# Second tiles' gate values moved from TensorE to VectorE, and first-pair operand splits moved behind the attention stage, in a fused attention and expert kernel

## What is computed

```
# 1 chunked attention: 8 heads of 64, chunks of 32 queries, each over 8 memory keys + up to 56 keys around it
a   = softmax(q_c @ k_full.T / 8);  x = a @ v_full
# 2 channel mix, with x_prev the row before
xk  = mu_k * x + (1 - mu_k) * x_prev;   xr = mu_r * x + (1 - mu_r) * x_prev
x2  = sigmoid(xr @ w_r) * (relu(xk @ w_k) ** 2 @ w_v)          # w_k 512x1024, w_v 1024x512, w_r 512x512
# 3 experts: logits of 8 experts and one local gate, row by row
logits = x2 @ w_gate;  local = sigmoid(x2 @ w_local)
e      = argmax(logits[s]) if s == 0 or local[s] < 0.5 else e of the row before
out[s] = softmax(logits[s])[e] * (relu(x2[s] @ w1[e]) @ w2[e])
```

## Time and profile before

| what | value |
|---|---|
| runs | 488.22, 488.89, 490.28 us, median 488.89 |
| profiled execution | 489.2 us, its span 487.6 us |
| mean granted TensorE clock | 0.945 |
| TensorE busy | 444.6 us (91%) |
| VectorE busy | 263.6 us (54%) |
| ScalarE busy | 222.2 us (46%) |
| attention stage | 0 to 74.56 us |
| six mix pairs | 74.56 to 261.4 us |
| rest of the routing | 261.4 to 283.4 us |
| expert slots | 283.4 to 487.6 us |

### The profile page before, as it was taken

How to read it: one execution, slowest core, us unless ns; L and a number is a source line. 1 busy time by engine, 2 the same in 40 slices (tenths; PEclk the granted TensorE clock), 3 DMA queues, 4 the chain that set the end, 5 groups by cost and what they waited for, 6 DMA issues and landing times.

```text
span 487.6 us, 9976 instructions
## 1 busy us (share of the span) xinstructions
PE 444.6 (91%) x3792; PEld 370.1 (76%) x3792; DVE 263.6 (54%) x596; ACT 222.2 (46%) x332; POOL 52.8 (11%) x70
## 2 busy tenths in 40 slices
PE   2686769999999999999999879999999999999991
PEld 2564558889898898988987667787777777777771
DVE  3577882355634656448494557223822374746851
ACT  1446652633636446354591145223622373727740
POOL 0001000000010100101001211112111111111110
PEclk9958557999999999999999989999999999999997
DMA  8889749825072270630911189311740166565610
GB/s 314 335 302 396 267 160 356 337 118 230 0 286 107 86 302 1 272 117 33 340 39 45 58 301 410 117 43 33 232 181 28 44 200 224 188 219 164 240 29 11
DMA packets 23729, 87.34 MB, mean 179 GB/s; under 512 B 3151, under 2 KB 3279, under 8 KB 23697
## 3 DMA queue, kind: packets, MB, share of 16 engines
q1 hardware_dynamic: 18048, 70.87, 39.4%
q0 software_dynamic: 5360, 16.04, 9.8%
q10 hardware_dynamic: 288, 0.02, 0.0%
HBM read 55.34 MB, written 32.62 MB: 180 GB/s over the span
## 4 chain that ended last, share of the span: by engine, by line
PE 82%; DMA 6%; DVE 4%; issue 3%; ACT 1%; POOL 0%; SPq 0%; POOLq 0%; ACTq 0%; DVEq 0%
PE PS L592 18%; PE PS L609 18%; PE PS L465 15%; PE PS L498 14%; PE PS L481 7%; PE PS L600 3%; PE PS L519 2%; PE PS L577 2%; DMA RAW<-wmix 1%; DMA VV<-tiles 1%; DMA QK<-tiles 1%; PE PS L418 1%; PE PS L509 1%; DMA CO<-consts 1%; PE PS L429 1%
## 5 line engine op out<-in xcount | busy, mean ns | idle before, releaser
L1100 DVE TENSOR_TENSOR EL<-ERAW,EH 128x1024 fp32r<-128x1024 f32 x56 | 66.5, 1217 | 2.7 <-ACT EH L797 2.6
L797 ACT ACTIVATE EH<-ERAW 128x1024 fp32r<-128x1024 f32 x56 | 57.6, 1056 | 11.3 <-PE PS L609 8.8
L465 PE MATMUL PS<-XHI,WHI 128*128 128x256 f32 x192 | 56.3, 293 | 0.9 <-issue 0.9
L1168 DVE TENSOR_TENSOR HL<-PS,HH 128x512 fp32r<-128x512 f32 x32 | 22.0, 690 | 64.8 <-ACT HH L811 64.8
L465 PE MATMUL PS<-XHI,WLO 128*128 128x256 f32 x192 | 54.8, 285 | 0.0
L465 PE MATMUL PS<-XLO,WHI 128*128 128x256 f32 x192 | 54.7, 285 | 0.0
L592 PE MATMUL PS<-EH,XSH 128*128 128x512 f32 x128 | 52.7, 412 | 1.4 <-DVE XSL L1106 1.4
L609 PE MATMUL PS<-EH,HH 128*128 128x512 f32 x120 | 51.0, 425 | 1.5 <-DVE EL L1100 0.6
L592 PE MATMUL PS<-EL,XSH 128*128 128x512 f32 x128 | 51.4, 401 | 0.0
L592 PE MATMUL PS<-EH,XSL 128*128 128x512 f32 x128 | 51.2, 400 | 0.0
L609 PE MATMUL PS<-EH,HL 128*128 128x512 f32 x120 | 47.3, 394 | 0.0
(11 more groups left out here) (157 smaller groups left out, 826.2 us busy)
## 6 DMA issues: line engine op xcount, KB each, us to landing
ERAW<-wexp SPq DMA_DIRECT2D x56, 512.0 KB, 5.7
expert_rows<-ZR SPq DMA_DIRECT2D x6, 4112.0 KB, 13.8
QK<-tiles SPq DMA_DIRECT2D x12, 768.0 KB, 6.8
VV<-tiles SPq DMA_DIRECT2D x12, 520.0 KB, 6.2
RAW<-wmix POOLq DMA_DIRECT2D x10, 512.0 KB, 6.0
XR<-expert_rows POOLq DMA_DIRECT2D x17, 257.0 KB, 3.2
CO<-consts SPq DMA_DIRECT2D x1, 340.0 KB, 6.2
rows_out<-OSB,OIDX POOLq DMA_INDIRECT x16, 5.3
```

Of the source, the lines that this page charges most:

```text
L465: last = nc.tensor.matmul(PS[q % 2][:, half * 256:half * 256 + 256], w[:, c:c + P], x[:, k, :], start=n == 0, stop=n == 11)
L797: nc.scalar.activation(expert_part(EH1, EH2, w, c), ERAW[c][:], ACT.Copy).then_inc(ehi_done, 1)
L1100: nc.vector.tensor_tensor(expert_part(EL1, EL2, w, c), ERAW[c][:], expert_part(EH1, EH2, w, c).bitcast(F32), ALU.subtract).then_inc(elo_do ...
L1168: nc.vector.tensor_tensor(HL[:, 4 * part:4 * part + 4, :].rearrange("p k n -> p (k n)"), PS[2 + part][:, :], HH[:, 4 * part:4 * part + 4, ...
```

## The change

Five things change.

1. The gate values (8 logits and the local gate) of the second tile of pairs 0 to 4 no longer come from TensorE. The nine weight columns are laid out as rows on the host (`wrows`), loaded once and copied to all partitions (`WGB`, nine tiles of 128 x 512), and VectorE's `products(p, part)` makes nine products with a sum over the row, three in each of three parts: before `squared(g, 0)`, before `squared(g, 1)` and before `squared(g, 2)`. TensorE loses four transposes and eight passes of `logits` in each of the pairs 1 to 5, ScalarE one `x2_out`, VectorE one `logits_out`. The last tile, t = 11, stays on TensorE.
2. Of the ten weight chunks 0 to 5 are split in the tiles 2, 3, 4, 5, 7 and 9 (`CHUNK_AT`), and chunks 6 to 9 (`w_v`) in pair 0, one behind each `relu_square` and `squared`. The load of chunk 6 waits for the values of tile 9.
3. Kind 1 of pair 0's inputs is built and split in `mix(0)`: `mix_scaled` and `mix_full` before the first `relu_square` and `squared`, `mix_hi` and `mix_lo` behind it.
4. SyncE's queue: the nine `WGB` loads stand behind the wait for all ten chunks and ahead of the zero writes, and the first expert's loads also wait until all of pair 4's products are made (`logit_evac` at 11), since `WGB` and `JUNK` lie in memory that is used again.
5. In `mix(5)` VectorE's `gated(5, 0)` stands ahead of `lo(5)`, `x_lo(0)` and `lo(6)`, no longer behind them.

```diff
+CHUNK_AT = {2: 0, 3: 1, 4: 2, 5: 3, 7: 4, 9: 5}
...
+        top[0] = inner + 2 * W2
+        JUNK = [X2T[1][:].rearrange("p k n -> p (k n)"), place("JUNK1", [P, D])[:]]
+        WGB = [place(f"WGB{e}", [P, D], at=(ring + KT * XTW + e * D if e < 4 else whi + N1 * CH1 + (e - 4) * D
+                                            if e < NE else wlo + N1 * CH1 + 2 * XGW + 4)) for e in range(NE + 1)]
... SyncE
+            sp.wait_ge(pv_done, NT)
+            sp.wait_ge(xt_done, NT)
             sp.wait_ge(wlo_done, N1)
+            for e in range(NE + 1):
+                sp.dma_start(WGB[e][:], wrows[e:e + 1, :].to_broadcast([P, D])).then_inc(wgb_loaded, 16)
...
             sp.wait_ge(xf_done[1], NPAIR)
+            sp.wait_ge(logit_evac, NT - 1)
             for c in SPLIT0:
                 expert_load(x, c)
... TensorE, mix
                 up(g, 0, first)
                 if not first:
-                    logits(2 * g - 2, 0, g - 1)
-                    x2_transposed(2 * g - 1, 1 if odd else 3, False)
+                    logits(2 * g - 2, g - 1, 0, g - 1)
                 up(g, 1, first)
-                if not first:
-                    logits(2 * g - 1, 1, g - 1)
... ScalarE
-                if t >= 2:
-                    weight_hi(t - 2)
-                if t in (6, 7):
-                    mix_scaled(0, t - 6, True)
-                if t in (8, 9):
-                    mix_hi(0, t - 8, True)
+                if t in CHUNK_AT:
+                    weight_hi(CHUNK_AT[t])
+                if t == 6:
+                    mix_scaled(0, 0, True)
+                if t == 8:
+                    mix_hi(0, 0, True)
...
             def mix(g, first, last):
-                if not first:
-                    x2_out(2 * g - 2, 0)
+                if first:
+                    mix_scaled(0, 1, True)
+                else:
+                    x2_out(g - 1, 0)
                 relu_square(g, 0, first)
-                if not first:
-                    x2_out(2 * g - 1, 1)
+                if first:
+                    mix_hi(0, 1, True)
+                    weight_hi(len(CHUNK_AT))
                 for q in range(1, 4):
                     relu_square(g, q, first)
+                    if first:
+                        weight_hi(len(CHUNK_AT) + q)
... VectorE (the attention tiles as on ScalarE)
+            def products(p, part):
+
+                t = 2 * p + 1
+                dve.wait_ge(wgb_loaded, 16 * (NE + 1))
+                dve.wait_ge(x2_done, t + 1)
+                for e in range(3 * part, 3 * part + 3):
+                    n = p * (NE + 1) + e
+                    if n >= 2:
+                        dve.wait_ge(product_done, n - 1)
+                    last = nc.vector.scalar_tensor_tensor(JUNK[n % 2], X2F[:, t % 4, 0:D], 1.0, WGB[e][:], ALU.mult,
+                                                          ALU.mult, accum_out=LG[:, t, e:e + 1])
+                    last.then_inc(product_done, 1)
+                if part == 2:
+                    dve.wait_ge(product_done, (p + 1) * (NE + 1))
+                    dve.sem_inc(logit_evac, 1)
...
+                if first:
+                    mix_full(0, 1, True)
+                else:
+                    products(p, 0)
                 squared(g, 0, first)
-                if not first:
-                    logits_out(2 * p)
+                if first:
+                    mix_lo(0, 1, True)
+                    weight_lo(len(CHUNK_AT))
+                else:
+                    logits_out(2 * p, p)
+                    products(p, 1)
                 squared(g, 1, first)
-                if not first:
-                    logits_out(2 * p + 1)
+                if first:
+                    weight_lo(len(CHUNK_AT) + 1)
+                else:
+                    products(p, 2)
                 squared(g, 2, first)
                 if first:
+                    weight_lo(len(CHUNK_AT) + 2)
...
                 squared(g, 3, first)
+                if first:
+                    weight_lo(len(CHUNK_AT) + 3)
...
+                if last:
+                    gated(g, 0, False)
                 lo(5)
                 if last:
                     x_lo(0, PS[1])
                     lo(6)
-                gated(g, 0, first)
+                else:
+                    gated(g, 0, first)
... GpSimd
+                if n == len(CHUNK_AT):
+                    pool.wait_ge(pv_done, NT - 2)
                 pool.dma_start(RAW[n % 2][:], wmix[:, n * CH1:(n + 1) * CH1]).then_inc(raw_loaded[n % 2], 16)
```

More of the change, by code:

```diff
@@ L54, with moe_program @@
 C_NF, C_POS, C_EXP, C_SLOT, CW = 508, 520, 584, 648, 808
+CHUNK_AT = {2: 0, 3: 1, 4: 2, 5: 3, 7: 4, 9: 5}
 SLAB = 52800
 FRESH_AT = -1.5 * 2.0 ** -23
-def moe_program(nc, tiles, wmix, mus, wgate, wexp, consts, out):
+def moe_program(nc, tiles, wmix, mus, wgate, wrows, wexp, consts, out):
     ctx = ExitStack()
@@ L219, in moe_program @@
         x2_done = sem("x2_done")
+        wgb_loaded = sem("wgb_loaded")
+        product_done = sem("product_done")
         x2t_done = sem("x2t_done")
@@ L501, in down, with x2_transposed @@
                     last.then_inc(down_done, 1)
-            def x2_transposed(t, at, first):
+            def x2_transposed(t, n, at, first):
                 pe.wait_ge(x2_done, t + 1)
                 if not first:
-                    pe.wait_ge(x2t_evac, t)
+                    pe.wait_ge(x2t_evac, n)
                 for k in range(KT):
@@ L511, in x2_transposed, with logits @@
                 last.then_inc(x2t_done, 1)
-            def logits(t, u, pairs):
-                pe.wait_ge(x2t_evac, t + 1)
+            def logits(t, n, u, pairs):
+                pe.wait_ge(x2t_evac, n + 1)
                 pe.wait_ge(logit_evac, t + 1)
@@ L561, in mix @@
                 if last:
-                    x2_transposed(2 * g, 2, False)
+                    x2_transposed(2 * g, g, 2, False)
                     down(g, 1, first, range(12, 18))
-                    logits(2 * g, 0, g)
+                    logits(2 * g, g, 0, g)
                     down(g, 1, first, range(18, 24))
@@ L567, in mix @@
                     down(g, 1, first, range(12, 24))
-                    x2_transposed(2 * g, 2 if odd else 0, first)
+                    x2_transposed(2 * g, g, 2 if odd else 0, first)
             def x_slot(s, bank):
@@ L630, in _ @@
             h_passes(0, 0, range(3))
-            x2_transposed(NT - 1, 3, False)
+            x2_transposed(NT - 1, NPAIR, 3, False)
             h_passes(0, 0, range(3, 7))
-            logits(NT - 1, 1, NPAIR - 1)
+            logits(NT - 1, NPAIR, 1, NPAIR - 1)
             h_passes(0, 0, range(7, 12)).then_inc(h_done, 1)
@@ L783, in sigmoid, with x2_out @@
                 nc.scalar.activation(SG[u][:], PS[2 + u][:, :], ACT.Sigmoid).then_inc(sig_done, 1)
-            def x2_out(t, u):
-                act.wait_ge(x2t_done, t + 1)
-                act.wait_ge(logit_done, t + 1)
+            def x2_out(n, u):
+                act.wait_ge(x2t_done, n + 1)
+                if u:
+                    act.wait_ge(logit_evac, NT - 1)
+                act.wait_ge(logit_done, n + 2)
                 nc.scalar.activation(X2T[u][:].rearrange("p k n -> p (k n)"), PS[6][:, :],
@@ L849, in _ @@
                 mix(g, g == 0, g == NPAIR - 1)
-            x2_out(NT - 2, 0)
-            x2_out(NT - 1, 1)
+            x2_out(NPAIR - 1, 0)
+            x2_out(NPAIR, 1)
             route_exps(NPAIR - 1)
@@ L967, in attention @@
                 normed(t, u, t < 2)
[L968 to L973, removed]
+                if t in CHUNK_AT:
+                    weight_lo(CHUNK_AT[t])
+                if t == 6:
+                    mix_full(0, 0, True)
+                if t == 8:
+                    mix_lo(0, 0, True)
             dve.wait_ge(const_in, 48)
@@ L1001, in squared, with logits_out @@
                                         ALU.subtract).then_inc(klo_done, 1)
-            def logits_out(t):
-                dve.wait_ge(logit_done, t + 3)
+            def products(p, part):
[12 more added lines that the diff above has]
+                    dve.sem_inc(logit_evac, 1)
+            def logits_out(t, n):
+                dve.wait_ge(logit_done, n + 3)
                 nc.vector.tensor_copy(LG[:, ds(t, 1), :].rearrange("p a n -> p (a n)"),
@@ L1011, in gated @@
                 dve.wait_ge(sig_done, t + 1)
-                if not first:
-                    dve.wait_ge(x2t_done, t - 1)
                 if g >= 2:
+                    if u == 0:
+                        dve.wait_ge(x2t_done, g - 1)
                     dve.wait_ge(rows_scattered, 32 * (g - 1))
@@ L1159, in mix @@
                 if last:
-                    logits_out(2 * g)
+                    logits_out(2 * g, g)
                 gated(g, 1, first)
@@ L1179, in _ @@
             tail = NPAIR - 1
-            logits_out(NT - 1)
+            logits_out(NT - 1, NPAIR)
             flags(tail)
@@ L1438 @@
```

(1 more changed line is left out.)

## The result

Four runs of the changed kernel took 481.45, 482.31, 482.78 and 483.42 us, median 482.54, against 488.79 for the kernel before: a ratio of 0.9866 with a 95% interval of 0.9836 to 0.9896. It is faster, by about half of what was forecast (476.6, range 472.5 to 482.0); the median lies just above the range. The profiled execution took 482.78, with a span of 481.2 us.

What follows compares the result with a forecast made beforehand. It took the mix pairs as bound by TensorE and attention by VectorE and ScalarE alternating. Terms -6.0 - 2.1 + 0.4 - 5.1 (pairs 1 to 4) + 0.5 = -12.3 took profiled 489.2 to 476.9, median 476.6; range 472.5 to 482.0.

Steps and rivals of the forecast that it cites:

- Attention: Attention stage: fewer splits there start the first `up` earlier, -4.7 us, and a risen clock gives -1.3 more, so -6.0.
- The ring: VectorE and ScalarE alternating in attention, some 6.6 us from tile 6 to 7; without `weight_hi` tile 6 loses 1.05 us.
- Rival 4: Attention: transfers take the gain, the tile period stays 5.5 us, -2 in place of -8.1, total 482.7; chance 0.07.
- the term for the clock: End of attention: the clock rises at about 58 us, before pair 0, and shortens six later steps, -1.3 us.
- Clock in pair 0: Pair 0: if the risen clock holds, `up` takes 11.4 us and not 13.5, -2.1 us.
- Rival 1: Attention and pair 0: the clock stays low until pair 0 as before, total 479.6; chance 0.25.
- Waits for RAW in pair 0: Pair 0: chunk 8's reload completes KLO at about 17.5 us, `down(0, 0)` would start at 17.1, +0.4 us.
- WGB loads and zero writes: Pair 0: nine loads land 8 to 9 us after issue, before needed, and later zero writes cost nothing: 0 us.
- Rival 3: Pair 1: WGB loads land late and hold VectorE's squares, total about 498, slower than before; chance 0.02.
- the sentence on the flag DMAs: Pair 0: zero writes may slow its small flag DMAs, for which VectorE has about 4 us in hand; taken as 0.
- Rival 2: VectorE's products in the pairs run at half rate, 1.25 us each, total 483.8; chance 0.08.
- Pair 5: Pair 5: expert loads 8 us later hold ScalarE and what follows, +0.5 us in place of -1.28.

Runs made afterwards that it cites:

- zero writes later: Changed kernel with each zero write after the first waiting for an earlier pair's state column to land: 478.57 us, ratio 0.9787 to the kernel before.
- load order: Changed kernel with the first expert's chunks loaded and split in the order 0, 1, 2, 3, 6, 7, 4, 5: 477.60 us, ratio 0.9759 to the kernel before.
- queue windows: Changed kernel with the new expert chunk order and zero writes placed to avoid flag DMAs and expert loads: 477.34 us, ratio 0.9752 to the kernel before.
- the filler: Changed kernel with extra unused identity matmuls in TensorE's gaps in attention and ahead of pair 0: 482.36 us, ratio 0.9846 to the kernel before.
- windows, less filler: The queue windows kernel with fewer extra identity matmuls than the filler: 474.55 us, ratio 0.9695 to the kernel before.
- larger filler: The filler's full set of extra matmuls, on the changed kernel (482.36 us) and on it with later zero writes and new expert load order (481.01 us).

## Why the prediction was wrong, step by step

**What bounds the kernel: right.** Pairs 2 to 4 lost 1.28 to 1.30 us each, the two pieces of the earlier trace rows.

**Attention, -6.0 forecast, -4.54 measured.** The ring shrank as worked out: tile 6 began at 44.09 instead of 43.25, tile 7 at 49.52, tile 8 at 53.84, tile 9 at 58.23, steps of 5.43, 4.32 and 4.39 where 5.55, 4.4 and 4.4 were forecast. Rival 4 (tiles stay at 5.5 us because of the transfers) fell with that. Two things make the miss of 1.5. The first is no step of the prediction: tile 6 started 0.84 later, in code that the change doesn't touch; over the twelve profiles it begins between 42.66 and 45.44. The second is the term for the clock. From tile 9 to the first `up` I had 12.2 us at the low clock and 1.3 less with the clock up; measured were 11.79, so the clock gave 0.4, since it was down again from 62 us. Three profiles of the same code in which it stood at 0.91 to 1.00 at 66 to 68 us (zero writes later, load order, queue windows) took 11.06, 10.80 and 11.10 there, about what I had forecast. That the stage came near the -4.7 without the clock is luck: the late start (0.8) cancels what the ring (0.2) and the clock (0.4) gave beyond it.

**Clock in pair 0, -2.1 forecast, +0.73 measured: the step that failed, and the largest miss.** "If it also holds into pair 0" was taken as given once the clock had risen. It rose earlier than I said, and then TensorE was idle more and the clock fell, as it had after 44 us in the kernel before, which the prediction does not use; it takes from that trace only the rise near 34 us. The cost is shown by the filler: pair 0 at 28.3 against 30.9. Without filler no profile of this code reached 28.3: pair 0 took 29.6 to 31.0, according to when the clock came back, between 72 and 76 us. Rival 1 named the low clock, but from one that never rises, and its 479.6 missed by 2.9.

**Waits for RAW in pair 0, +0.4 forecast, 0 measured.** The test is the last kernel (windows, less filler), where `up` ran at full clock. ScalarE waited 1.96 us for chunk 8, yet the last KLO ended at 84.58 us and `down` began at 85.86, 1.3 us later. I had the KLO at 17.5 us into the pair and it was at 15.8: chunk 6 was split at 7.8, as worked out, but chunk 8 could be used 4.2 us after that, where I had taken 6.0 from the median of loads that had run beside others.

**WGB loads and zero writes, 0 forecast: the loads right, the zero writes the second step that failed.** Nine loads landed 3.3 to 7.2 us after issue, and VectorE's first product waited for none; the last had landed 1 us before it. Rival 3 fell. But the sentence on the flag DMAs ("VectorE has about 4 us in hand") failed twice: they were slowed from 1.9 to 5.9 us, two of them in series, 8 us together; and the engine that then stood still was TensorE, of which the sentence says nothing. It is ready for the ranks at its 13th pass of `down(1, 1)`, 26.1 us into the pair when nothing holds it, had some 6.8 us in hand, and waited. That cost 1.35 us in pair 1, shown by moving the zero writes.

**The products, 0.72 us each forecast, 0.61 measured; hidden, right.** Rival 2 fell: at 688 ns the form with a row sum from two float32 SBUF inputs runs at the rate of the `tensor_tensor` of the earlier trace rows, 692. The Trainium skill ("Vector Engine (DVE) Microarchitecture Reference", section 7) says that its throughput is halved when both SBUF sources are other than bf16; this trace disagrees. The Trainium skill ("VectorE: DVE Perf Modes", the section on two Vector instructions with no wait between them) says that an op which writes out its accumulator is two instructions; the trace agrees, with the second at 81 ns, inside the pitch.

**Pair 5, +0.5 forecast, +1.21 measured: mechanism right, size off by 0.7.** The last product ended 10.7 us into the pair, as forecast, ScalarE stood 3.7 us at its first split (forecast 4.6) and 1.1 at the next two, and TensorE waited for `place_rows` 1.5 us where I had 1. Which term lacks the 0.7 stays open: other profiles with the old load order and part 5 lie 0.6 to 1.6 above the kernel before in this stretch. The load order with its later split gives back 2.9 us.

**What stays open.** The place where attention ends differs by 1.8 us between profiles that run the same code there (68.55 to 70.37 without filler), and pair 0 by 1.4, so a difference of under some 0.5% between the totals of two of these kernels says little by itself. The scatter goes with the clock: of the six runs of the queue-windows kernel the one with the highest mean granted clock (0.976) took 473.94 us, the one with the lowest (0.959) 478.79. And the expert slots took 204.2 to 204.6 us in some profiles and 203.3 to 203.6 in others. In four of the five shorter ones a row load of some 6 us stands in the chain and in none of the longer, so that load is not what makes the others longer. The cause stays open.

## What to carry to other kernels

When a wait is shortened or a transfer moved in a queue, list the small transfers that will now run beside it and what the second and third engine behind them need; a DMA of 2 KB took three times as long beside one of 4 MB. When engines are in order, the first late instruction counts by what stands behind it, not by the work it does. A clock that has risen can't be credited with staying up: look in the profile of the kernel before for places where it rose and fell again, and at what the engine did between. And when an edit is to be credited with a gain, compare stage by stage: more than half of the difference that the later zero writes seemed to make lay in stages that they could not touch.

## What the runs showed of the hardware that was not expected

A DMA of 1 or 2 KB that landed in 1.9 us when no zero write ran took 5.6 to 6.8 us in pair 1 beside zero writes of 4,112 KB on another queue. The first expert's loads of 512 KB do the same: in pair 5 of the changed kernel `FL` took 6.3 us, where it had taken 3.8 in the kernel before. With filler the granted clock stood at 1.00 in every stretch of 2 us from 30 us on, although TensorE was busy only 0.84 of 2 us in one of them with the larger filler, and 0.68 with the smaller:

```profile
50.00:52.00 2.00, 0.68 (x54) 0.52 (x33) 1.67 (x7) 1.39 (x2) 0.00 (x0) 1.00 1.03 421
```

Without filler three stretches in a row with 1.09, 1.04 and 0.69 stood ahead of the fall. So one idle stretch alone did not bring it down; where the limit lies is not shown. A full clock in attention is not shown to make attention shorter: the first `up` came at 71.42 and 71.46 us with the larger filler and at 68.83 with the smaller, against 68.55 to 70.37 without.
